# Unit-stride columns for attention's rows, the update in two 64-row tiles, and level 5's second chunk one quadrant lower

## What is computed

```python
# attention: q, k, v, f_logit are [4 batches, 8 heads, 768 tokens, 48]
f = 1 / (1 + exp(-f_logit))
for t in range(768):
    state = f[t][:, None] * state + k[t] (outer) v[t]     # 48 x 48 for each head
    y[t] = q[t] @ state
x = y with the heads side by side                         # [3072 tokens, 384]
h = x @ w_in;  g = h * sigmoid(1.702 * h);  x2 = g @ w_out     # 384 -> 2048 -> 384
p = domain_probs / sum;  out = sum_e p[:, e] * (relu(x2 @ w1[e]) @ w2[e])   # 4 experts
```

## Time and profile before

| | us |
|---|---|
| median of 3 runs | 1356.08 (1355.3 to 1356.3) |
| the profiled execution | 1355.08 |
| its span in the trace | 1353.3 |
| of it, PE busy | 1326.8 |
| DVE, POOL, ACT busy | 890.9, 629.0, 568.4 |

### The profile page before, as it was taken

The page is one execution under the profiler, slowest core; times in us unless marked ns, Lnnn a source line. Parts: engine busy times, 40 slices in busy tenths (PEclk is TensorE's granted clock), DMA queues, the critical chain, the costliest instruction groups (busy, mean ns, idle before and its releaser), DMA issues.

```text
span 1353.3 us, 26477 instructions
## 1 busy us (share of the span) xinstructions
PE 1326.8 (98%) x10837; PEld 1233.1 (91%) x10837; DVE 890.9 (66%) x1354; ACT 568.4 (42%) x975; POOL 629.0 (46%) x721
## 2 busy tenths in 40 slices
PE   6899999999999999999999999999999999999999
PEld 5788999999999999998999999999999999999998
DVE  8786858475858583566666666666666666666666
ACT  5673636363636363453233333333323433334341
POOL 8786747484747573655121212112212544443330
PEclk9999999999999999999999999999999999999999
DMA  9636252525252521220101101010001112222211
GB/s 157 135 74 104 60 84 63 86 61 85 62 88 59 87 59 40 79 74 24 35 13 35 36 13 35 12 36 24 25 24 59 36 47 70 71 70 75 66 35 47
DMA packets 240200, 79.34 MB, mean 59 GB/s; under 512 B 189136, under 2 KB 238544, under 8 KB 240080
## 3 DMA queue, kind: packets, MB, share of 16 engines
q1 hardware_dynamic: 201680, 74.11, 23.0%
q10 hardware_dynamic: 38400, 3.55, 2.2%
HBM read 67.83 MB, written 9.78 MB: 57 GB/s over the span
## 4 chain that ended last, share of the span: by engine, by line
PE 89%; ACT 3%; DVE 2%; issue 2%; POOL 2%; SPq 1%; DMA 1%; ACTq 0%; DVEq 0%; POOLq 0%
PE bank L1917 10%; PE bank L1915 10%; PE bank L1916 10%; PE bank L1851 9%; PE bank L1852 9%; PE bank L1850 9%; PE bank L1823 5%; PE bank L1582 4%; PE bank L1825 4%; PE bank L1824 4%; PE bank L1580 4%; PE bank L1581 4%; PE bank L1635 3%; PE bank L1591 1%; PE bank L1781 1%
## 5 line engine op out<-in xcount | busy, mean ns | idle before, releaser
L1529 DVE SCALAR_TENSOR_TENSOR acc<-bank,p_n,acc 128x384 f32<-128x384 f32 x384 | 235.0, 612 | 67.9 <-PE bank L1917 62.9
L1917 PE MATMUL bank<-w_h,h_l 128*128 128x384 f32 x768 | 257.3, 335 | 0.0
L1915 PE MATMUL bank<-w_h,h_h 128*128 128x384 f32 x768 | 257.2, 335 | 0.0
L1916 PE MATMUL bank<-w_l,h_h 128*128 128x384 f32 x768 | 257.0, 335 | 0.0
L1513 DVE TENSOR_TENSOR bank<-bank,x_copy 128x512 f32<-128x512 f32 x192 | 124.5, 694 | 165.9 <-ACT x_copy L1187 102.4
L836 POOL TENSOR_TENSOR g_l<-sig,g_h 128x384 fp32r<-128x384 f32 x128 | 157.7, 1232 | 157.4 <-ACT g_h L1090 157.3
L1852 PE MATMUL bank<-xs,we_l 128*128 128x512 f32 x528 | 206.5, 391 | 0.0
L1851 PE MATMUL bank<-xs,we_h 128*128 128x512 f32 x528 | 206.4, 391 | 0.0
L1850 PE MATMUL bank<-xs,we_h 128*128 128x512 f32 x528 | 205.5, 389 | 0.7 <-issue 0.7
L888 POOL TENSOR_TENSOR we_l<-we_raw,we_h 128x384 fp32r<-128x384 f32 x96 | 96.5, 1033 | 215.4 <-ACT we_h L1155 215.3
L1187 ACT ACTIVATE x_copy<-bank 128x512 f32<-128x512 f32 x144 | 86.1, 598 | 222.1 <-PE bank L1852 221.7
(11 more groups left out here) (156 smaller groups left out, 2387.2 us busy)
## 6 DMA issues: line engine op xcount, KB each, us to landing
we_raw<-in_moe_w SPq DMA_DIRECT2D x32, 384.0 KB, 3.9
w_raw<-in_moe_w SPq DMA_DIRECT2D x32, 384.0 KB, 3.3
v_sb<-in_v SPq DMA_DIRECT2D x48, 96.0 KB, 2.7
x_dram<-work SPq DMA_DIRECT2D x8, 576.0 KB, 4.7
x_raw<-x_dram SPq DMA_DIRECT2D x12, 384.0 KB, 4.4
f_raw<-in_f_logit SPq DMA_DIRECT2D x56, 72.0 KB, 2.1
q_raw<-in_q SPq DMA_DIRECT2D x56, 72.0 KB, 2.0
k_raw<-in_k SPq DMA_DIRECT2D x56, 72.0 KB, 2.1
```

The lines of the kernel that those rows point to most:

```text
L1529: dve.scalar_tensor_tensor(acc[:, pr * TT + i, :], y_bank[y % 3][:, 0:DM], p_n[:, col:col + 1], acc[:, pr * TT + i, :], ALU.mult, ALU.add) ...
L1915: pe.matmul(dst, hh, wh, start=f == 0, stop=False)
L1916: pe.matmul(dst, hh, wl, start=False, stop=False)
L1917: last = pe.matmul(dst, hl, wh, start=False, stop=f == 1)
```

## The change

- v's row becomes [head 0 | 16 zeros | head 1 | 16 zeros] of 128 elements. Row 32 r + p of block m is now row 96 r + 32 m + p of x. Block 0 holds only elements of a pair's first head, block 2 only of its second, and block 1 the last 16 of the one and the first 16 of the other. `TILE_PARTS` lists the four parts that are left; `y` takes 16 products in place of 24. v's, the state's and y_rows' columns are read with stride one.
- w_in's rows are loaded in the same order, four runs of 32 rows in place of every third row. In half 0 `y_rows` is written in that order too.
- `update` of halves 1 to 7: eight products of 64 weights columns and 48 moving ones, at array columns 0 and 64, one for a head, in place of four.
- Level 5 of halves 1 to 7: chunk 1's products come out 32 partitions lower, at 32 and 96, and alternate with chunk 0's pair by pair; chunk 2 follows as before. ACT reads chunk 1's scores 32 partitions lower than it writes them.

```diff
-    VW = 3 * D
+    VW = 2 * GAP
...
-    win_v = w_in.rearrange("(p k) n -> k p n", p=P)
+    win_v = w_in.rearrange("(r k p) n -> k r p n", r=PAIRS, k=KT)
...
+    TILE_PARTS = [(0, 0, 0), (1, 0, SQ), (1, 1, D), (2, 1, D + SQ)]
+
+    def v_columns(c, r, first):
+
+        return v_sb[:, c, r, first:first + SQ]
...
+        return state[:, r, m * SQ:(m + 1) * SQ]
...
+                down = SQ if L == SQUARE and i == 1 and not fine(n) else 0
                 for lo in range(0, P, 2 * m):
                     done = act.activation(scores_of(i, L, n)[lo:lo + m, :, lo + m:lo + 2 * m],
-                                          by_head[lo:lo + m, :, lo // 2:lo // 2 + m], ACT.Copy)
+                                          by_head[lo + down:lo + down + m, :, lo // 2:lo // 2 + m], ACT.Copy)
...
+            def square_level(n):
+                first, second, third = (level_unit[SQUARE] + i for i in range(CH))
+                bank_free(first, n)
+                bank_free(second, n)
...
+                for r in range(PAIRS):
+                    cols = slice(r * P, (r + 1) * P)
+                    upper = tiles_of_level(SQUARE, ring[first % 3][:, cols], r * CH)
+                    if r == PAIRS - 1:
+                        upper.then_inc(unit_ready, 1)
+                    lower = tiles_of_level(SQUARE, ring[second % 3][:, cols], r * CH + 1, SQ)
+                lower.then_inc(unit_ready, 1)
+                bank_free(third, n)
+                for r in range(PAIRS):
+                    last = tiles_of_level(SQUARE, ring[third % 3][:, r * P:(r + 1) * P], r * CH + 2)
+                last.then_inc(unit_ready, 1)
...
-                for m in range(KT):
-                    for j in range(2):
-                        for r in range(PAIRS):
-                            last = add(r, m, v_columns(c, 2 * r + j, m), scores_T[:, c, 2 * r + j, :],
-                                       m == 0 and j == 0, m == KT - 1 and j == 1 and not from_state)
+                for m, j, first in TILE_PARTS:
+                    for r in range(PAIRS):
+                        last = add(r, m, v_columns(c, r, first), scores_T[:, c, 2 * r + j, :],
+                                   m == 0, m == KT - 1 and not from_state)
...
+                        for j in range(2):
+                            lo, h = GAP * j, 2 * r + j
+                            last = pe.matmul(ring[u % 3][lo:lo + GAP, h * D:(h + 1) * D],
+                                             k_rows[:, h * GAP:(h + 1) * GAP], v_head(c, h), start=True, stop=True,
+                                             tile_position=(0, lo))
```

More of the change, by code:

```diff
@@ L562, in load_piece @@
                 dst = stages[stage_of[i]][:, 0:width]
-                src = win_v[o // FF, :, o % FF:o % FF + width] if which == "in" else wout_v[:, o // DM, :]
+                src = win_v[o // FF, :, :, o % FF:o % FF + width] if which == "in" else wout_v[:, o // DM, :]
                 sp.dma_start(dst, src).then_inc(w_loaded[stage_of[i]], 16)
@@ L1394, in step @@
                     dve.wait_ge(v_diag_ready, c + 1)
-                    dve.tensor_tensor(y_rows[:, :], ring[u % 3][:, 0:DM], v_diag[:, :], ALU.add)\
+                    by_tile = y_rows[:, :].rearrange("p (k r x) -> p r k x", k=KT, r=PAIRS)
+                    dve.tensor_tensor(by_tile, ring[u % 3][:, 0:DM].rearrange("p (r k x) -> p r k x", k=KT, r=PAIRS),
+                                      v_diag[:, :].rearrange("p (r k x) -> p r k x", k=KT, r=PAIRS), ALU.add)\
                         .then_inc(read_by["dve"], counts(c, a))
@@ L1590, in tiles_of_level @@
                     own = slice(lo // 2, (lo + width) // 2)
-                    last = pe.matmul(into[lo:lo + width - m, :, own], k_T[:, x * P + lo:x * P + lo + width - m],
-                                     q_split[:, x, :, own], start=True, stop=True, tile_position=(0, lo))
-                return last
+                    to = lo + down
+                    last = pe.matmul(into[to:to + width - m, :, own], k_T[:, x * P + lo:x * P + lo + width - m],
+                                     q_split[:, x, :, own], start=True, stop=True, tile_position=(0, to))
+                return last
+            def square_level(n):
+                first, second, third = (level_unit[SQUARE] + i for i in range(CH))
+                bank_free(first, n)
+                bank_free(second, n)
+                pe.wait_ge(split_ready, (n * (LEVELS - FIRST) + SQUARE - FIRST + 1) * 2 * CH)
+                pe.wait_ge(kg_ready, (n * LEVELS + SQUARE) * CH)
+                for r in range(PAIRS):
[9 more added lines that the diff above has]
+                last.then_inc(unit_ready, 1)
             def last_level(n):
@@ L1688, in step @@
                         last_level(n)
+                        return
+                    if L == SQUARE and not fine(n):
+                        square_level(n)
                         return
@@ L1779, in step @@
                     for r in range(PAIRS):
-                        into = ring[u % 3][0:GAP + D, r * 2 * D:(r + 1) * 2 * D].rearrange("p (j d) -> p j d", j=2)
-                        last = pe.matmul(into, k_rows[:, r * P:r * P + GAP + D], v_heads(c)[:, r, :, :],
-                                         start=True, stop=True)
+                        if fine(n):
+                            into = ring[u % 3][0:GAP + D, r * 2 * D:(r + 1) * 2 * D].rearrange("p (j d) -> p j d", j=2)
+                            last = pe.matmul(into, k_rows[:, r * P:r * P + GAP + D], v_heads(c)[:, r, :, :],
+                                             start=True, stop=True)
+                            continue
+                        for j in range(2):
[3 more added lines that the diff above has]
+                                             tile_position=(0, lo))
                     last.then_inc(unit_ready, counts(c + 1, a) + (c == CH - 1 and not fine(n)))
@@ L1789, in step @@
                     for m in range(KT):
-                        last = pe.transpose(ring[u % 3][:, m * P:(m + 1) * P], y_rows[:, m::KT], ident[:, :])
+                        last = pe.transpose(ring[u % 3][:, m * P:(m + 1) * P], y_rows[:, m * P:(m + 1) * P], ident[:, :])
                     last.then_inc(unit_ready, 1)
```

16 lines of the change are left out of this document (6 added, 10 removed).

## The result

The changed kernel is slower, where a clear gain was forecast. In five pairs of runs on one chip it took 1364.04 us in the median (1362.57 to 1364.49), the kernel before 1356.30 (1355.30 to 1358.00): a ratio of 1.0053, 95% interval 1.0038 to 1.0068. The profiled execution took 1364.04 us with a span of 1362.3, 9.0 us more than the span of before.

What follows compares the result with a forecast made beforehand. PE was taken as the bound, busy 1326.8 of 1353.3 us. Savings in y and the update, kept half by half, summed to 9.3 us (level 5 and the rest 0), taking the median from 1356.08 to 1346.8; range 1343.0 to 1352.5.

Steps and rivals of the forecast that it cites:

- The rest: w_in's reordered load and half 0's y_rows: same rows, lengths and elements, so 0, give or take 0.3 us.
- Rival D: Update: switching between the two array halves stops PE at each record; 8 us more, 1364 us; 4%.
- y with the state: y's products: each chunk's y loses 16 records at 27.1 ns, 0.433 us, with or without the state's part.
- An update to the second product behind it: Update call, halves 1 to 7: 0.88 us from its start, where it was 1.06, saving 0.18 a call.
- Level 5: Halves 1 to 7: 0.45 us shorter in each, 3.1 us of PE time, all lost in level 6's wait.
- PE's wait at level 6: PE's wait for q_split in halves 1 to 7: grows from 4.1 to about 7.2 us in total.
- ACT's squares: ACT's six copies in level 5, read 32 partitions away: still 0.385 us each, 2.31 us together.
- D's bound: Update's step per record: the slower case decides from 83 ns on; the forecast took 29.8 ns.
- The halves: PE's saving kept per half: 0, 1.84, 0.75, 1.84, 1.66, 1.54 and 1.66 us for halves 1 to 7, sum 9.3.
- Half 1 gives nothing: End of half 1 hangs on a chain without PE, up to POOL's g_l; PE waits its saving out: 0.
- The cap: Half 3: DVE's transpose of q needs loads landing at 264.5 us, standing at 265.20; at most 0.75 us kept.
- this wait in half 6: layer_out(11) waits for POOL's g_l: 0.61 us saved ahead, 0.3 can be kept, so half 6 gives 1.54.

Runs made afterwards that it cites:

- new_rows_before: The kernel before with only w_in's pieces read in the new order of rows, x keeping its old rows (timing only); 1371.80 us, ratio 1.0110.
- old_rows_after: The changed kernel with only w_in's pieces read in the old order of rows, x keeping its new rows (timing only); 1348.13 us, ratio 0.9937.
- quads_first: grouped7_v_late with w_in's pieces for half 1 and one of w_out issued behind the quads of f_logit, q and k; 1350.24 us, ratio 0.9945.
- old_rows_y48: old_rows_after with y's first product of each pair issued three times over, so 48 records a chunk, 72 with the state's; 1354.88 us, ratio 0.9984.
- grouped_no_level5: Changed kernel with w_in loaded 32 rows outermost, partly in grouped DMAs, one stage buffer fewer, and level 5 as in the kernel before; 1352.16 us, ratio 0.9968.
- grouped7_v_late: grouped7 with the DMAs of v and the probabilities issued behind the sixteen f_logit blocks on SP's queue; 1353.43 us, ratio 0.9974.
- grouped7: Changed kernel with w_in loaded 32 rows outermost, its first six pieces grouped into 8 DMAs, all seven stage buffers kept; 1353.71 us, ratio 0.9980.

## Where the prediction was right and where it was wrong

**The step that failed** is "The rest": w_in's load "has the same number of rows of the same length, in other order ... I take 0, give or take 0.3 us". In the traces of the kernel before and of new_rows_before it costs 13.9 us in half 0 and 3.4 more by the end of half 1, where ACT waits 4.6 us for f's quads and PE 1.9 and 1.7 us behind it; the medians are 15 us apart, because the one profiled execution lies 1.2 us below its median and the other 1.7 above. What the load lost is not bytes but engines: 102 GB/s on what amounts to four of them. I compared packets and bytes, and never looked at the outermost dimension of the source. The bound of 0.3 us had no row under it. Rows for it were there: SPq issues from 9.5 to 53 us with hardly a break, and ACT's sigmoid of the f blocks began as soon as they had landed even before (0.2 us of wait). No rival had this case either. Rival D names 1364 us, but by a mechanism that isn't there; that the number is met is chance.

**The sizes of the parts** were right. From first to last start in the same block: y with the state 1.920 to 1.463 us, without it 1.265 to 0.808, so 0.457 a chunk for a forecast of 0.433. An update to the second product behind it 0.88 us, for 0.88; to the first product behind it, it saves 0.206 a call. Level 5 gets 0.446 us shorter, for 0.45, and PE's wait at level 6 grows to 7.4 us, for 7.2. ACT's squares, read 32 partitions away, take 2.32 us for 2.31. D's bound, a record from 83 ns on, is far off: 15 steps in 0.450 us are 30 ns each, for a forecast of 29.8.

**The halves** are best compared where nothing is late, in old_rows_after. PE's gain on the kernel before, from chunk 0's y of one half to that of the next, read from the starts of its blocks:

| half | 1 | 2 | 3 | 4 | 5 | 6 | 7 | sum |
|---|---|---|---|---|---|---|---|---|
| forecast, us | 0 | 1.84 | 0.75 | 1.84 | 1.66 | 1.54 | 1.66 | 9.3 |
| old_rows_after | -0.44 | 0.65 | 2.19 | 1.61 | 1.27 | 0.63 | 1.64 | 7.6 |
| quads_first | -0.53 | 1.47 | 1.72 | 1.34 | 1.43 | 0.75 | 1.77 | 8.0 |

The sum was 1.3 to 1.7 us too high, and its shares were off. Half 1 gives nothing, as forecast. Half 3 was capped at 0.75 by the load of q and gave 1.7 to 2.2. The cap had two faults. The 2.3 us to landing run from the start of an issue and I counted them from its end: the last load of q landed at 264.01 us (issued at 261.70) and not at 264.5, so the room before the transpose was 1.2 us and not 0.7. And the load moved: counted from chunk 0's y it landed 1.0 us earlier in old_rows_after and in the changed kernel than before, largely because the sixteen issues of f ahead of it took 9.28 and 9.70 us and not 10.41. I took that duration as fixed. The limit itself is real: in the changed kernel DVE's transpose of q starts at 279.13 us, 0.14 after the landing.

Halves 2, 4 and 6 lose in two places. One is g_l: after an early chunk 0 layer_out(11) comes before POOL is done. In the changed kernel PE waits 1.3, 0.9 and 0.8 us for it in these halves and nowhere in halves 3, 5 and 7; in old_rows_after it is 1.7 in half 2 and nothing in 4 and 6. I had seen this wait in half 6 alone, since in the kernel before POOL's duration there ranges from 1.0 to 4.4 us with the phase of DVE's copies, and I took each half's own phase as fixed. The other is the start of the next pass, of which the prediction had no term: within its first four slots PE gives back 0.4, 0.4 and 0.5 us behind halves 2, 4 and 6 in the changed kernel, and 0.4, 0.5 and 1.0 in old_rows_after, where `hidden` meets DVE's product of `sig`, which stands behind the transposes of q and k. In half 6 of old_rows_after ACT's `sig` is done at 466.07 us, DVE comes to its product at 466.90, as the transposes end, and PE starts again at 467.48.

With w_in's load in the old order, old_rows_after's 1348.1 us is 1.3 us from the forecast of 1346.8.

## What to carry to other kernels

When a change alters the order in which a transfer walks its source, write out both access patterns and look at the outermost sizes, not only at bytes and row lengths: four DMAs with 32 rows outermost cost a queue more issues and still beat one with 4. A queue that issues without a break is a resource like an engine; a transfer that gets slower shows up in the instructions of its neighbours, and small DMAs added ahead of an urgent one can give back what they win. A wait between two free-running engines has a phase, so what one half shows of it is not to be taken as fixed for that half.

## What the runs showed of the hardware that I had not expected

- A load of 256 KB in rows of 2 KB whose outermost source dimension is 4 keeps the DMA engines two to three tenths busy and moves 102 GB/s, where 128 outermost reaches 388; while it runs, each later issue on the same queue takes some 2 us and not 0.46 (w_in) or 0.84 (v). A packet of 2 KB takes as long as before, 83 ns for 86.
- Going from y's 32-column tiles into the update costs 0.202 us from the last start to the first, whether the update has the full form or two 64-column tiles. Leaving it costs 0.152 us from the tiled form and 0.045 from the full one. The Trainium skill (TensorEngine Tiling (Array Packing), Key Properties) has a drain at each change of mode; the trace agrees that there is one, and finds none dearer for a third form.
- POOL's subtraction of 128 x 384 takes 1.0 us alone and up to 4.5 us beside three copy_predicated of DVE, which then lose nothing themselves (3.85 and 3.84 us). In another phase it is the copies that pay: in half 3 of the changed kernel the subtraction takes 1.79 us and they take 4.68.
- In three profiles (old_rows_y48, grouped_no_level5, grouped7_v_late) the clock granted to TensorE fell between 76 and 86 us, with PE busy 15.5, 14.4 and 13.1 of the 16 us ahead of that (in old_rows_after, without a fall, 14.5): 0.83 in the mean, so part of it at 1.2 GHz and not 2.4. In old_rows_y48 nine products of layer_out took 2.72 us from first to last start and not 1.50. Windows of old_rows_y48 and of old_rows_after:

```profile
76.00:86.00 10.00, 7.24 (x124) 6.87 (x124) 9.36 (x13) 4.29 (x8) 6.48 (x5) 0.83 0.32 98
```

```profile
76.00:86.00 10.00, 10.00 (x239) 9.40 (x237) 9.97 (x13) 5.85 (x11) 10.00 (x9) 1.00 0.34 101
```

  PE falls back by 4.2 us there in old_rows_y48; 2.1 are left at the end of half 1, with half 1's own longer y among them. What sets it off was not settled. The clock granted over a whole execution goes with its time, though: the six of old_rows_after lie in its order, from 1345.97 us at 0.999 to 1351.08 at 0.995. It isn't all of the scatter: of grouped7's executions, two at 0.996 took 1352.00 and 1356.64.
